# Two mixture-of-experts layers behind an attention: the second x gets a buffer of its own, two groups of transposes move into the first two products, and VectorE makes the token numbers

## The chip, the cores and the metric

The kernel runs on one core of a Trainium2 chip. The metric is the device time of one execution in microseconds (us), and lower is better. TensorE (PE in the profile; PEld are its weight loads) does matrix products, VectorE (DVE), ScalarE (ACT) and GpSimd (POOL) work on elements, SyncE (SP) issues most of the DMAs, and GpSimd issues those that gather or scatter rows by index.

## The reference, cut to what matters

An attention with pooled queries gives 1152 tokens of 512 numbers. They pass two mixture-of-experts layers. Each layer picks one of 8 experts for each token and computes

```python
e_idx = np.argmax(x @ w_gate, axis=1)
gate_w = softmax(x @ w_gate)[arange(N), e_idx]
for e in range(8):
    mask = e_idx == e                       # layer 1: at most `capacity` tokens of an expert
    h = np.maximum(x[mask] @ w1[e], 0.0)    # 512 -> 1024
    y[mask] = gate_w[mask, None] * (h @ w2[e])   # 1024 -> 512
# layer 1: out = y.   layer 2: out = x + y, for tokens with x @ w_skip > 0 only; the others keep x
```

## The kernel before, in words

The code calls the layers m = 0 and m = 1; here they are layer 1 and layer 2. After the attention the x of all tokens lies in device memory (`x_dram`).

**Routing.** VectorE finds each token's expert and its place in a list sorted by expert, cut into tiles of 128 places. The upper and the lower 64 places of a tile may belong to different experts. To turn the places into row indices, VectorE makes `r_tile` (which tile, line 1460) and `r_place` (which place inside, line 1465, three token groups at a time), GpSimd multiplies `r_tile` by the token numbers into `r_ids` (line 651), and TensorE sums the products of `r_place` and `r_ids` (line 892). VectorE writes the result as `rows_in` (line 1473).

**The tiles.** Tile t goes through these steps:

- GpSimd gathers the 128 rows of x into `xraw` (`load_x`, line 601);
- TensorE turns them with 4 transposes (`turn_x`, line 918), ScalarE copies the result to `XT` in two halves (`copy_xt`, line 1154);
- TensorE makes the first product, `hidden_product`: for each of the 4 chunks c of 128 inputs, 4 rows; a row is one matmul of 64 tokens by the expert in the ring `w1ring` (line 931) and, beside it in the other half of the array, one of 64 tokens by `wright` (line 933). `wright` is a copy of the right half's expert, made in four parts by `fill_right` (line 319);
- ScalarE writes relu times gate to `hid` (`relu`, line 1161), TensorE turns it with 8 transposes (`turn_hidden`, also line 918), ScalarE copies to `HT` (line 1169);
- TensorE makes the second product, `y_product`, also 16 rows. VectorE copies the result out, and GpSimd scatters it (line 630).

TensorE's order is written out by hand. A `step(t)` is: first product of t, second product of t - 1, turn x of t + 1, turn hidden of t. In step 0 there is no second product of a tile before, so nothing but the turns stands between first product 0 and first product 1. Here the text calls that stretch the handover. First product 1 writes the same PSUM banks as first product 0, so it waits for relu 0 (`relu_ready`). VectorE refills `wright` for tile 1 when first product 0 is done (`hidden_done`). There are 10 tiles in layer 1 and 9 in layer 2. `keep_busy` are matmuls whose result nobody reads.

Semaphores count what is done: `x_loaded` is raised by 16 by each gather, `x_turned` by 1 for each turned x, `xt_ready` by 1 for each half of `XT`, `w1_right` by 1 for each part of `wright`.

## Time and profile before

| | us |
|---|---|
| median of 3 runs | 610.27 (609.8 to 610.33) |
| the profiled execution | 610.99 |
| its span (first to last instruction) | 608.0 |
| TensorE busy | 589.3 |
| VectorE busy | 313.5 |
| ScalarE busy | 267.1 |
| GpSimd busy | 187.5 |
| attention, from the start to | about 272 |
| routing of layer 1, then its products | 272 to 287.3, then to 442.9 |
| routing of layer 2, then its products | 446 to 460.6, then to 601.2 |

All times below are counted from the start of the span. A row of the timeline shows the start, the duration, the engine, the line, the operation and its operands, and in brackets how long the engine was idle before it and what ended that. When one row holds several instructions ("x4"), the duration is that of all of them.

### The profile page before, as it was taken

The page shows a single profiled execution, that of the slowest core. Times are in us where ns is not written, and L with a number is a line of the kernel's source. Part 1 is how long each engine was busy: PE and PEld are TensorE (multiplying, and loading weights), DVE is VectorE, ACT ScalarE, POOL GpSimd, SP SyncE. Part 2 cuts the span into 40 slices and gives each one's busy share as a digit, 9 for nine tenths or more (in the row PEclk, how much of TensorE's full clock was granted, in tenths as well). Part 3 has the DMA queues.
Part 4 walks back from the last instruction along what each step waited for, and adds up shares of the span by engine and source line. Part 5 has one row for each costly group of instructions (what it writes and reads, how often), then busy time and mean ns, then how long its engine had stood idle before and what let it go on. Part 6 is the DMA issues. An engine that isn't in the chain of part 4 may idle for free.

```text
span 608.0 us, 12473 instructions
## 1 busy us (share of the span) xinstructions
PE 589.3 (97%) x3739; PEld 351.6 (58%) x3740; DVE 313.5 (52%) x658; ACT 267.1 (44%) x440; POOL 187.5 (31%) x164
## 2 busy tenths in 40 slices
PE   8899999999999999999999999999999999999994
PEld 7678787777777877768333333333485333333333
DVE  5457565657566666657324872876674211311111
ACT  4556565556566565530144444444102444444410
POOL 4686534435261900001111121122112022222223
PEclk9999999999999999999999999999999999999998
DMA  8979917262622054002999787890856798951111
GB/s 202 291 176 259 207 41 159 56 142 44 156 47 58 1 160 174 21 12 58 391 415 352 319 315 283 327 322 26 308 183 227 266 314 326 322 180 44 45 52 62
DMA packets 42636, 111.60 MB, mean 184 GB/s; under 512 B 16020, under 2 KB 16020, under 8 KB 41536
## 3 DMA queue, kind: packets, MB, share of 16 engines
q1 hardware_dynamic: 38528, 99.03, 51.4%
q0 software_dynamic: 4080, 12.22, 5.8%
q8 instruction: 15, 0.25, 0.2%
q14 instruction: 13, 0.11, 0.1%
HBM read 102.68 MB, written 12.06 MB: 189 GB/s over the span
## 4 chain that ended last, share of the span: by engine, by line
PE 88%; DVE 4%; issue 3%; DMA 2%; ACT 2%; POOL 1%; DVEq 0%; POOLq 0%; SPq 0%; ACTq 0%
PE psum L931 40%; PE psum L700 15%; PE psum L714 12%; PE psum L748 10%; PE psum L918 4%; PE psum L781 3%; PE psum L760 1%; PE psum L744 1%; DVE probs L1210 1%; ACT probs L1047 1%; DMA qraw<-in_q_dram 1%; PE psum L933 1%; PE psum L839 1%; DMA xraw<-moe_in,rows_in 1%; DMA xraw<-moe_in,idx_x 1%
## 5 line engine op out<-in xcount | busy, mean ns | idle before, releaser
L931 PE MATMUL psum<-w1ring,XT 128*64 x304 | 134.5, 595 | 0.8 <-ACT XT L1154 0.4
L931 PE MATMUL psum<-w2ring,HT 128*64 x336 | 133.7, 552 | 1.6 <-DVE wright L319 1.6
L933 PE MATMUL psum<-wright,XT 128*64 128x512 f32 x304 | 134.5, 595 | 0.0
L933 PE MATMUL psum<-wright,HT 128*64 128x512 f32 (+1 forms) x336 | 133.7, 552 | 0.0
L1210 DVE TENSOR_SCALAR_CACHE_REDUCE probs<-psum 128x1152 f32<-128x1152 f32 x72 | 97.6, 1357 | 62.5 <-PE psum L700 62.5
L1047 ACT ACTIVATE probs<-probs,nmax 128x1152 f32<-128x1152 f32 x72 | 90.7, 1260 | 45.6 <-DVE probs L1210 45.6
L700 PE MATMUL psum<-KT,QT 128*128 128x384 f32 x480 | 101.9, 350 | 3.0 <-DVE probs L1210 1.8
L931 PEld LDWEIGHTS psum<-w2ring,HT 128*64 128x64 f32 x336 | 45.9, 137 | 83.6 <-issue 79.5
L700 PEld LDWEIGHTS psum<-KT,QT 128*128 128x128 f32 x480 | 80.2, 188 | 15.0 <-issue 7.9
L931 PEld LDWEIGHTS psum<-w1ring,XT 128*64 128x64 f32 x304 | 40.1, 137 | 79.8 <-issue 79.8
L714 PE MATMUL psum<-ident,probs 128*128 128x128 f32 x648 | 82.0, 275 | 1.1 <-ACT probs L1047 0.6
L714 PEld LDWEIGHTS psum<-ident,probs 128*128 128x128 f32 x648 | 72.7, 140 | 9.2 <-issue 3.7
L1161 ACT ACTIVATE hid<-psum,slot_gate 128x1024 f32<-128x1024 f32 x19 | 21.2, 1114 | 125.1 <-PE psum L933 125.1
L1054 ACT COPY PT<-psum 128x512 f32<-128x512 f32 x88 | 48.4, 588 | 60.3 <-PE psum L714 60.3
L319 DVE COPY wright<-w2ring 128x1024 f32 x76 | 50.5, 715 | 23.3 <-DMA w2ring<-in_moe_w_dram 23.3
L748 PE MATMUL psum<-PT,V 128*64 128x512 f32 x256 | 62.2, 605 | 0.0
L319 ACT COPY wright<-w1ring 128x1024 f32 x60 | 58.1, 1041 | 0.0
L1389 DVE CUSTOM_DVE_ANT_0 psum<-ysb,wnext 128x512 f32<-128x512 f32 x81 | 52.9, 723 | 3.9 <-DMA wnext<-in_next_w_dram 3.9
L1382 DVE TENSOR_TENSOR orow<-psum,res 128x512 f32<-128x512 f32 x8 | 5.5, 692 | 89.3 <-PE psum L933 89.3
L933 PEld LDWEIGHTS psum<-wright,HT 128*64 128x64 f32 x336 | 45.9, 137 | 0.0
L331 POOL CAST KT<-kraw 128x2304 fp32r<-128x2304 f32 x7 | 14.7, 2107 | 87.2 <-PE psum L700 81.2
L1217 DVE COPY PT<-psum 128x512 f32<-128x512 f32 x56 | 36.4, 687 | 8.3 <-PE psum L714 8.3
(166 smaller groups left out, 602.2 us busy)
## 6 DMA issues: line engine op xcount, KB each, us to landing
w1ring<-in_moe_w_dram SPq DMA_DIRECT2D x64, 512.0 KB, 6.2
w2ring<-in_moe_w_dram SPq DMA_DIRECT2D x64, 512.0 KB
qraw<-in_q_dram SPq DMA_DIRECT2D x30, 288.0 KB, 10.1
kraw<-in_k_dram SPq DMA_DIRECT2D x14, 576.0 KB, 9.1
V<-in_v_dram SPq DMA_DIRECT2D x8, 576.0 KB, 4.0
moe_in<-zero SPq DMA_DIRECT2D x9, 256.0 KB, 3.1
wnext<-in_next_w_dram SPq DMA_DIRECT2D x1, 2304.0 KB, 16.0
out_dram<-moe_in SPq DMA_DIRECT2D x1, 2304.0 KB
```

Of the source, the lines that this page charges most:

```text
L319: copy(wright[k][:, part * PIECE:(part + 1) * PIECE], piece_of(k, slot, part).rearrange("p o f -> p (o f)")).then_inc(filled, 1)
L700: mm = pe.matmul(dst, QT[par][:, piece, q0:q0 + P], KT[par][:, b * S + c * KB:b * S + (c + 1) * KB], start=(i == 0), stop=(i == 2 * len(pa ...
L714: mm = pe.transpose(bank(T_BANK + place % 3)[:, i * P:(i + 1) * P], src, ident[:])
L748: mm = pe.matmul(psum[rows, PV_BANK, :], V[par][:, b * KT_N + j, :], PT[:, j, :], start=(j < 2), stop=False, skip_group_check=True)
L918: return pe.matmul(place[:, chunk * P:(chunk + 1) * P], src, ident[:], is_transpose=True, start=first, stop=False, skip_group_check=True)
L931: pe.matmul(psum[0:GRAIN, b, 0:width], lhs[:, c * P:c * P + GRAIN], left, start=first, stop=last, skip_group_check=True)
L933: return pe.matmul(psum[GRAIN:P, b, 0:width], lhs[:, c * P + GRAIN:(c + 1) * P], wright[k][:, cols], start=first, stop=last, skip_group_ch ...
L1047: nc.scalar.activation(probs[:, t, :], probs[:, t, :], ACT.Exp, bias=nmax[:, t:t + 1], scale=-1.0, accum_out=den[:, t:t + 1]).then_inc(pro ...
L1054: nc.scalar.copy(dst, bank(T_BANK + place % 3, cols)).then_inc(turned_by_act, 1)
L1210: nc.vector.tensor_scalar(probs[:, t, :].rearrange("p (c k) -> p c k", c=3), scores_in(h, t), -SCALE, None, ALU.mult, ALU.min, accum_out=n ...
L1217: nc.vector.tensor_copy(dst, bank(T_BANK + place % 3, cols)).then_inc(turned_by_dve, 1)
L1389: nc.vector.tensor_tensor_reduce(out=bank(JUNK_BANK + e % 2), in0=ysb[:], in1=wnext[:, e, :], scale=1.0, scalar=0.0, op0=ALU.mult, op1=ALU ...
```

## The change

Three things change.

1. `xsecond` is a new buffer for the x of tile 1, with its own semaphore. GpSimd issues its gather right behind that of tile 0. TensorE turns it inside first product 0, behind chunk 1, into the bank of the second product (`turn_second`). VectorE copies it to `XT`, between the parts of `wright`; ScalarE did it before.
2. The 8 transposes of `hid` of tile 0 stand inside first product 1, behind chunk 1, and no longer ahead of it.
3. VectorE makes `r_ids` for the token numbers, between `r_tile` and `r_place`; GpSimd did it before.

The core of the diff:

```diff
+        xsecond = sb_in(moe, "xsecond", [P, DM])
...
+        second_loaded_ = [sem(f"second_loaded_{m}") for m in range(2)]
...
                 def load_x(t, count):
 
-                    wait(pool, x_turned, t)
+                    if not isinstance(t, int) or t > 1:
+                        pool.wait_ge(x_turned, 1 if isinstance(t, int) and t == 2 else t)
                     settle()
                     index = rows_in[m][:, t:t + 1] if isinstance(t, int) else idx_x[:]
+                    into, loaded = (xsecond, second_loaded_[m]) if isinstance(t, int) and t == 1 else (xraw, x_loaded)
...
-                n = ROUTED[m]
-                token = token_id if m == 0 else slot_token
-                pool.wait_ge(tile_ready, m + 1)
-                nc.gpsimd.tensor_tensor(r_ids[:, 0, 0:n, :], r_tile[:, 0:n],
-                                        token[:, 0:n].unsqueeze(2).to_broadcast([P, n, NSLOT]), ALU.mult
-                                        ).then_inc(ids_ready, 1)
                 if m == 0:
                     pool.wait_ge(x_stored, 16 * 4 * H)
                 pool.wait_ge(rows_in_ready, m + 1)
                 load_x(0, 0)
+                load_x(1, 0)
                 pool.wait_ge(tables_ready, m + 1)
                 rest = pool.value_load(tab_n[m][0:1, 0:1], min_val=0, max_val=NSLOT - 2)
-                load_x(1, 0)
                 step(0, first=True)
...
+                def turn_second():
+                    pe.wait_ge(second_loaded_[m], 16)
+                    for c in range(DC):
+                        mm = turn_into(bank(Y_BANK), xsecond[:, c * P:(c + 1) * P], c, c == 0)
+                    mm.then_inc(x_turned, 1)
+
-                def hidden_product(t, place=None):
+                def hidden_product(t, place=None, between=None):
...
+                        if between and c == 1:
+                            between()
                     mm.then_inc(hidden_done, 1)
...
-                step(0, first=own)
-                step(1)
+                hidden_product(0, own, turn_second)
+                pe.wait_ge(gates_found, m + 1)
+                hidden_product(1, None, lambda: turn_hidden(0))
+                y_product(0)
+                turn_x(2)
+                turn_hidden(1)
...
-                    copy_xt(t + 1)
+                    if not isinstance(t, int):
+                        copy_xt(t + 1)
                     copy_hidden(t)
...
-                nc.vector.tensor_tensor(of(r_tile), per_tile(iota_slot, NSLOT), per_slot(r_which), ALU.is_equal
-                                        ).then_inc(tile_ready, 1)
+                tt(of(r_tile), per_tile(iota_slot, NSLOT), per_slot(r_which), ALU.is_equal)
+                token = token_id if m == 0 else slot_token
+                nc.vector.tensor_tensor(r_ids[:, 0, 0:n, :], of(r_tile), per_slot(token), ALU.mult).then_inc(ids_ready, 1)
...
                 dve.wait_ge(hidden_done_[m], START + 1)
-                fill_right(dve, nc.vector.tensor_copy, FIRST, m, *following, w1_right_[m])
+                dve.wait_ge(x_turned_[m], 2)
+                for i in range(2):
+                    cols = slice(i * DM // 2, (i + 1) * DM // 2)
+                    fill_right(dve, nc.vector.tensor_copy, FIRST, m, *following, w1_right_[m], (i,))
+                    nc.vector.tensor_copy(XT[:, cols], bank(Y_BANK)[:, cols]).then_inc(xt_ready_[m], 1)
+                fill_right(dve, nc.vector.tensor_copy, FIRST, m, *following, w1_right_[m], (2, 3))
```

On TensorE, this stood before between the last row of first product 0 and the first row of first product 1 (line 918 are the transposes, line 914 loads the expert's number of the next tile):

```order
L933 MATMUL psum<-wright,XT 64x512
L918 MATMUL psum<-ident,xraw 128x128 x4
L918 MATMUL psum<-ident,hid 128x128 x8
L914 TENSOR_LOAD tab_grain
L914 ISA x2
L946 ISA
L931 REGISTER_ALU
L931 ISA
L931 MATMUL psum<-w1ring,XT 64x512
```

This stands there in the changed kernel (its lines 912, 929, 931 and 950 are 914, 931, 933 and 946 of before):

```order
L931 MATMUL psum<-wright,XT 64x512
L912 TENSOR_LOAD tab_grain
L912 ISA x2
L950 ISA
L929 REGISTER_ALU
L929 ISA
L929 MATMUL psum<-w1ring,XT 64x512
```

Both groups of transposes have left the handover. Where they went reads like this. In the middle of first product 0, around its ninth row, TensorE had before

```order
L931 MATMUL psum<-w1ring,XT 64x512
L933 MATMUL psum<-wright,XT 64x512
L931 ISA
L931 MATMUL psum<-w1ring,XT 64x512
L933 MATMUL psum<-wright,XT 64x512
```

and has now

```order
L929 MATMUL psum<-w1ring,XT 64x512
L931 MATMUL psum<-wright,XT 64x512
L916 MATMUL psum<-ident,xsecond 128x128 x4
L929 ISA
L929 MATMUL psum<-w1ring,XT 64x512
L931 MATMUL psum<-wright,XT 64x512
```

The four transposes of the second x have come in between two rows. The eight of `hid` stand at the same place of first product 1.

On VectorE, at the refill of `wright` for tile 1, this stood before:

```order
L319 REGISTER_ALU
L319 ISA
L319 COPY wright<-w1ring 128x1024
L319 ISA
L319 COPY wright<-w1ring 128x1024
L319 ISA
L319 COPY wright<-w1ring 128x1024
```

and this stands there now:

```order
L321 REGISTER_ALU
L321 ISA
L321 COPY wright<-w1ring 128x1024
L1532 COPY XT<-psum 128x256
L321 ISA
L321 COPY wright<-w1ring 128x1024
L1532 COPY XT<-psum 128x256
L321 ISA
L321 COPY wright<-w1ring 128x1024
```

The first half of `XT` now follows the first part of `wright`, the second half the second part.

## Rows read from the trace of the kernel before

**Rows 1.** The page's chain of work that ended last, by engine.

```profile
PE 88%; DVE 4%; issue 3%; DMA 2%; ACT 2%; POOL 1%; DVEq 0%; POOLq 0%; SPq 0%; ACTq 0%
```

**Rows 2.** Timeline of the handover of layer 1 (start us, us, engine, line, operation).

```profile
293.82 0.59 PE L931 MATMUL psum<-w1ring,XT 128*64 x1
...
294.53 1.11 ACT L1161 ACTIVATE hid<-psum,slot_gate 128x1024 f32<-128x1024 f32 x1 [7.40 <-PE psum L933]
...
294.87 0.63 PE L918 MATMUL psum<-ident,xraw 128*128 128x128 f32 x4 [0.45 <-issue]
294.88 2.50 DVE L319 COPY wright<-w1ring 128x1024 f32 x4 [6.85 <-PE psum L933]
...
295.70 1.09 PE L918 MATMUL psum<-ident,hid 128*128 128x128 f32 x8 [0.20 <-ACT hid L1161]
...
297.07 0.64 PE L931 MATMUL psum<-w1ring,XT 128*64 x1 [0.28 <-issue]
```

**Rows 3.** Timeline of the handover of layer 2.

```profile
467.11 0.59 PE L931 MATMUL psum<-w1ring,XT 128*64 x1
...
467.83 1.11 ACT L1161 ACTIVATE hid<-psum,slot_gate 128x1024 f32<-128x1024 f32 x1 [7.38 <-PE psum L933]
...
468.18 2.50 DVE L319 COPY wright<-w1ring 128x1024 f32 x4 [6.37 <-PE psum L933]
...
468.99 1.09 PE L918 MATMUL psum<-ident,hid 128*128 128x128 f32 x8
...
470.19 0.64 PE L931 MATMUL psum<-w1ring,XT 128*64 x1
```

**Rows 4.** Timeline of TensorE between second product 0 and first product 2.

```profile
310.42 0.59 PE L931 MATMUL psum<-w2ring,HT 128*64 x1
...
310.95 0.66 PE L918 MATMUL psum<-ident,xraw 128*128 128x128 f32 x4
311.44 1.04 PE L918 MATMUL psum<-ident,hid 128*128 128x128 f32 x8
312.41 0.64 PE L931 MATMUL psum<-w1ring,XT 128*64 x1
...
312.89 0.59 PE L931 MATMUL psum<-w1ring,XT 128*64 x1
```

**Rows 5.** Timeline of VectorE in the attention: a copy out of PSUM.

```profile
271.50 0.43 DVE L1230 COPY OT<-psum 128x256 f32<-128x256 f32 x1 [0.54 <-PE psum L744]
```

**Rows 6.** Busy time, granted clock (PEclk) and DMA of the handover of layer 1.

```profile
294.40:297.05 2.65, 1.75 (x14) 1.27 (x12) 2.17 (x4) 2.36 (x5) 0.67 (x1) 1.00 0.99 368
```

**Rows 7.** Routing of layer 1: timeline, and durations (ns, min/median/max) of `r_place`.

```profile
277.73 0.29 DVE L1460 TENSOR_TENSOR r_tile<-iota_slot,r_which 128x126 f32<-128x126 f32 x1
278.19 0.55 POOL L651 TENSOR_TENSOR r_ids<-r_tile,token_id 128x126 fp32r<-128x126 f32 x1 [63.63 <-DVE r_tile L1460]
280.40 0.17 DVE L1473 TENSOR_SCALAR rows_in<-psum 128x14 int32<-128x14 f32 x1
...
L1465 DVE TENSOR_TENSOR r_place<-iota_p,r_inside x3: 545/550/755, 277.9 to 279.1; 128x384 fp32r<-128x384 f32 x3
```

**Rows 8.** The same in layer 2.

```profile
450.80 0.36 DVE L1460 TENSOR_TENSOR r_tile<-iota_slot,r_which 128x196 f32<-128x196 f32 x1
452.06 0.50 PE L892 MATMUL psum<-r_ids,r_place 128*128 128x14 f32 x3 [0.36 <-POOL r_ids L651]
454.52 0.17 DVE L1473 TENSOR_SCALAR rows_in<-psum 128x14 int32<-128x14 f32 x1 [0.81 <-PE psum L892]
...
L1465 DVE TENSOR_TENSOR r_place<-iota_p,r_inside x5: 411/546/876, 451.1 to 453.3; 128x384 fp32r<-128x384 f32 x4, 128x256 fp32r<-128x256 f32 x1
```

**Rows 9.** The first turns of x, and landing times of the gathers of 281 to 298 us.

```profile
285.79 0.65 PE L918 MATMUL psum<-ident,xraw 128*128 128x128 f32 x4 [1.29 <-DMA xraw<-moe_in,rows_in]
459.16 0.60 PE L918 MATMUL psum<-ident,xraw 128*128 128x128 f32 x4
...
DMA to landing us min/median/max: 4.1/7.2/7.4
```

More of the change, by code:

```diff
@@ L197, in build @@
         hot_ready, pos_ready, exp_ready, diff_ready = (sem(n) for n in ("hot_ready", "pos_ready", "exp_ready", "diff_ready"))
-        tile_ready, inside_ready, kept_ready = sem("tile_ready"), sem("inside_ready"), sem("kept_ready")
+        inside_ready, kept_ready = sem("inside_ready"), sem("kept_ready")
         active_ready, ot_part = sem("active_ready"), sem("ot_part")
         ylast_copied, last_logits = sem("ylast_copied"), sem("last_logits")
+        second_loaded_ = [sem(f"second_loaded_{m}") for m in range(2)]
         y_half_, orow_half = [sem(f"y_half_{m}") for m in range(2)], sem("orow_half")
@@ L313, in right_slot, with fill_right @@
             return expert, eng.snap(ring_slot(k, m, expert))
-        def fill_right(eng, copy, k, m, expert, slot, filled):
-            for part in range(PARTS):
+        def fill_right(eng, copy, k, m, expert, slot, filled, parts=range(PARTS)):
+            for part in parts:
                 eng.wait_ge(w_loaded[k][part], expert * 16 + (E * m + 1) * 16)
@@ L601, in load_x @@
                     nc.gpsimd.indirect_dma_start(
-                        out=xraw[:], out_offset=None, in_=x_dram[m],
+                        out=into[:], out_offset=None, in_=x_dram[m],
                         in_offset=bass.IndirectOffsetOnAxis(ap=index, axis=0),
-                        bounds_check=B * SQ - 1, oob_is_err=False).then_inc(x_loaded, 16)
+                        bounds_check=B * SQ - 1, oob_is_err=False).then_inc(loaded, 16)
                 def load_residual(t, count):
@@ L675, in _ @@
                     store_y(rest + 1, done + 1)
-                pool.wait_ge(x_loaded, rest * 16 + 64)
+                pool.wait_ge(x_loaded, rest * 16 + 48)
                 settle()
@@ L921, in turn_x @@
                 def turn_x(t):
-                    pe.wait_ge(x_loaded, 16 * t + 16)
+                    pe.wait_ge(x_loaded, 16 if isinstance(t, int) and t == 0 else 16 * t)
                     wait(pe, xt_ready, 2 * t)
@@ L1011, in next_logits, with step @@
                     mm.then_inc(lg_done, 1)
-                def step(t, first=None):
-                    hidden_product(t, first)
-                    if first:
-                        pe.wait_ge(gates_found, m + 1)
-                    else:
-                        y_product(t - 1)
+                def step(t):
+                    hidden_product(t)
+                    y_product(t - 1)
                     turn_x(t + 1)
@@ L1475, in _ @@
                 tt(r_gcut[:, 1, 0:n], of(gate), r_gcut[:, 0, 0:n].bitcast(F32), ALU.subtract)
-                dve.wait_ge(tile_ready, m + 1)
                 for i in range(2):
```

## The prediction, made before the changed kernel was run

> **What bounds the kernel now.** I read the page first, and there the chain of work that ended last: TensorE holds 88% of it [rows 1], and its busy time is 589.3 us of a span of 608.0 us. So an edit pays only where it takes TensorE's idle time away, and costs wherever it gives TensorE more to wait for. The timeline of the stretches that the change touches comes next. In the steady steps TensorE has no idle time: no row has a bracket [rows 4]. The two handovers, between first product 0 and first product 1 of each layer, do have some. There I count from T, the start of the last row of first product 0.
>
> In layer 1, T is 293.82 and the first row of product 1 starts at 297.07, 3.25 us later [rows 2]. In layer 2 it is 467.11 and 470.19, 3.08 us [rows 3]. Both end the same way: the last row ends at T + 0.6, relu 0 runs to T + 1.82 (294.53 + 1.11 - 293.82), the 8 transposes of `hid` follow it to T + 2.97, and product 1 starts 0.28 us (layer 1) or 0.11 us (layer 2) after them. The 4 transposes of x run while relu does, so they cost nothing there.
>
> The third place is the routing. In layer 1 the first turn of x waits 1.29 us for the gather [rows 9], so whatever delays `rows_in` delays everything behind it. In layer 2 the first turn has no idle time ahead of it [rows 9].
>
> **The change part by part.**
>
> *The transposes inside the products.* Their price is read where TensorE turns without waiting [rows 4]. Rows of a product follow each other every 0.43 us. The first transpose starts 0.53 us after the last row, 0.10 more than a row would; 4 transposes take 0.49 us (310.95 to 311.44), 8 take 0.97 us (311.44 to 312.41); the row behind starts the next one after 0.48 us, 0.05 more. So four inside a product cost 0.10 + 0.49 + 0.05 = 0.64 us, and eight 0.10 + 0.97 + 0.05 = 1.12 us. Together 1.76 us for a layer, all on the path, as a product has no gap to hide them in. The least they can cost is 12 x 0.122 = 1.46 us, if entering and leaving is free; in the other direction I allow 1.9 us, as a mixture of x and `w1ring` rows is not in the trace.
>
> *The handover without transposes.* What is left between the products is the longest of three waits. Relu 0 still has to end, at T + 1.82, since product 1 writes the banks that relu reads. The first part of `wright` has to be copied by VectorE, which starts at T + 1.06 (294.88 - 293.82; 1.07 in layer 2) and takes 2.50 / 4 = 0.63 us for a part. And the first half of `XT` now comes behind that part on VectorE. The copy of 128 x 256 numbers from PSUM took VectorE 0.43 us [rows 5], so it ends at T + 1.06 + 0.63 + 0.43 = T + 2.12. To the first row I add 0.2 us, between the 0.28 and the 0.11 above: T + 2.3. The bounds are T + 1.93 (relu ends last, and 0.11 behind it) and T + 2.7 (the second wait ahead of the copies and the registers of `fill_right` add as much again as the lag). So the handover shrinks from 3.25 to 2.3 us in layer 1 (-0.95) and from 3.08 to 2.3 us in layer 2 (-0.78). The second wait of VectorE, for `x_turned` 2, ends in the middle of product 0 and adds no delay; behind it are queued the parts of `wright` for both products, and TensorE waits for those. The two XT copies push the parts for second product 0 back by some 0.8 us; they are wanted only after the 16 rows of first product 1, 6.9 us, and that covers it. Part 1 of `wright` follows the first XT copy by 0.63 us, and TensorE wants it 4 rows, 1.7 us, later.
>
> The sum of these two is the point of this case: before, relu covered the four x transposes, and the handover held all twelve. Now the handover holds none, but relu and the copies are bare, and the transposes are paid in full elsewhere.
>
> *The gather of the second x.* It goes ahead of the wait for the tables and the register load on GpSimd, and raises a semaphore of its own, so SyncE, which starts the `w2ring` loads when `x_loaded` reaches 16, still waits for the first x alone. Issued about 1.3 us behind the first, it lands at the latest 7.4 us later [rows 9], at about 290.5; its turn stands behind 8 rows of product 0, at 287.4 + 3.4 = 290.8. So it costs nothing, and the gather of the third x takes its old place. On the first x, whose landing took 4.1 us, I count no delay; the bound is the 7.4 us that a gather took beside `w2ring` loads, 3.3 us more.
>
> *Token numbers on VectorE.* In layer 1 `r_ids` comes ahead of `r_place` and costs VectorE what `r_tile` of the same shape takes, 0.29 us, with 0.02 for the link. GpSimd's product ran from 278.19 to 278.74, beside the second `r_place`, and one of the three took 755 ns where the others took about 545 [rows 7]. That 0.21 us comes back. So `rows_in` moves by 0.31 - 0.21 = +0.10 us, and the first x with it; the bounds are -0.1 and +0.31. In layer 2 TensorE waited for GpSimd until 452.06 [rows 8]. Now the first `r_place` would start at 450.80 + 0.36 + 0.02 + 0.28 = 451.46 and take 546 ns: 452.01. So TensorE starts as before, and since VectorE waits for TensorE ahead of `rows_in` there, nothing changes: 0.
>
> The Trainium skill (GPSIMD Engine Reference, Specifications) says that GpSimd's access to SBUF is shared with VectorE, and that VectorE instructions with two SBUF inputs contend with it. The slow `r_place` of each layer, 755 and 876 ns [rows 7, 8], agrees. Without that rule the 0.21 us would be taken for noise, and the sum would be 0.2 us higher.
>
> *The sum.* 2 x 1.76 - 0.95 - 0.78 + 0.10 = +1.89 us. Behind the handovers TensorE goes on without idle time, so it reaches the end. The profiled execution would go from 610.99 (span 608.0 and 2.99 around it) to 612.88; it lies 0.72 us above the median of the runs, 610.27, which gives 612.2.
>
> **The rivals.**
>
> *A: relu bounds the handover, and the switches are free.* If VectorE's copies are done before relu, and entering and leaving a product with transposes costs nothing, a layer pays 1.46 + 1.93 against 3.25 or 3.08: +0.14 and +0.31, with routing at 0 some +0.5 us, 610.8. For it: relu's end at T + 1.82 is only 0.3 us from the copy's. Against it: VectorE started 0.35 us after ScalarE in both layers [rows 2, 3], and the 0.10 us ahead of the first transpose is in the trace [rows 4].
>
> *B: the transposes vanish inside the products (the other side).* The place is the same two products; the price of the twelve would be 0 in place of 1.76, because the page shows weight loads busy for only 58% of the span against TensorE's 97%, and transposes could use what the rows leave. Then the sum is 0.10 - 0.95 - 0.78 = -1.6 us, 608.6. It decides once the twelve cost less than 0.8 us. Against it: the same twelve moved the next row by 1.5 us in the steady steps, where nothing waited [rows 4].
>
> *C: the second gather delays the first.* Both go through the same queue. If the first x landed as late as one beside a weight load, that is +3.3 us in layer 1 and as much in layer 2, at the most 618.8. For it: TensorE does wait for that x [rows 9]. Against it: its data is under way before the second's rows can be, since the issue alone takes over 1 us.
>
> *D: the clock falls.* The granted clock was 1.00, that is 2.4 GHz, over the handover of layer 1, with its pauses and twelve transposes [rows 6]. The changed kernel has one pause of about 1.9 us in place of shorter ones. At 1.2 GHz the 16 rows of product 1 would take 6.9 us more in each layer: up to 626. Against it: nothing in the handovers before made it fall.
>
> **How the numbers follow.** The forecast has a chance of 0.66, A 0.20, B 0.07, C 0.05, D 0.02. The predicted time is 612.2 us. The forecast's own bounds: transposes 1.9, a start at T + 2.5 and routing +0.31 give +2.8, which is 613.0; to A it reaches down to 610.8. With a few tenths for the runs the range is 610.6 to 613.5. A run pair of this kernel can tell about 0.2% from no change, 1.2 us: faster is below 609.05, slower above 611.49. Slower is the forecast, C and D, 0.73; A is the same, 0.20; B is faster, 0.07.
>
> **What would show it.** In the profile of the changed kernel: ninth rows of first products 0 and 1 that start about 1.07 and 1.55 us after the eighth instead of 0.43; a handover of about 2.3 us from T, ended by VectorE's copy of `XT` and not by relu; no idle time ahead of the turn of `xsecond`; all `r_place` near 550 ns, and `rows_in` 0.1 us later in layer 1. A handover under 1.5 us, or inserted transposes under 0.8 us a layer, would make the forecast wrong in sign.

## The result, and the profile after

| | before | changed |
|---|---|---|
| median (us) | 610.03 (609.67 to 610.33, 4 runs) | 614.02 (613.5 to 614.75, 4 runs) |
| ratio, with its 95% interval | | 1.0064 [1.0053, 1.0076] |
| profiled execution, and its span | 610.99, 608.0 | 613.5, 611.7 |
| granted clock, mean of a run | 0.996 or more in the profiled execution and in all 90 runs made beside the experiments | 0.991 to 0.995 |

The change made the kernel 4.0 us slower, twice the forecast of 1.9, and outside the range. The span grew by 3.7 us.

The first view is the timeline of the changed kernel around the handover of layer 1. Lines have moved: the rows of a first product are now L929, the transposes L916, relu L1168, the copies of `wright` L321, the copies of `XT` L1532.

```profile
290.23 0.59 PE L929 MATMUL psum<-w1ring,XT 128*64 x1
...
290.76 0.65 PE L916 MATMUL psum<-ident,xsecond 128*128 128x128 f32 x4
...
291.35 0.64 PE L929 MATMUL psum<-w1ring,XT 128*64 x1
...
291.83 0.59 PE L929 MATMUL psum<-w1ring,XT 128*64 x1
...
294.40 0.59 PE L929 MATMUL psum<-w1ring,XT 128*64 x1
...
295.11 1.11 ACT L1168 ACTIVATE hid<-psum,slot_gate 128x1024 f32<-128x1024 f32 x1 [8.17 <-PE psum L931]
295.46 0.69 DVE L321 COPY wright<-w1ring 128x1024 f32 x1 [7.22 <-PE psum L931]
296.07 0.42 DVE L1532 COPY XT<-psum 128x256 f32<-128x256 f32 x1
...
296.95 0.64 PE L929 MATMUL psum<-w1ring,XT 128*64 x1 [1.95 <-DVE XT L1532]
...
298.29 1.06 PE L929 MATMUL psum<-w1ring,XT 128*64 x1
...
299.14 1.06 PE L929 MATMUL psum<-w1ring,XT 128*64 x1
```

This answers to [rows 2]. The handover runs from 294.40 to 296.95: 2.55 us, where it was 3.25. It is ended by VectorE's copy of `XT`, as forecast. No idle time stands ahead of the turn of `xsecond`, so its gather came in time. The first turn of x starts no later than before (below): rival C is out. The four transposes push the ninth row from 290.66 (0.43 behind the eighth) to 291.35, and the tenth follows 0.48 later: 1.12 + 0.48 - 0.86 = 0.74 us for the four. The last two rows show what the forecast had set aside: rows of product 1 that last 1.06 us in place of 0.59 and follow each other every 0.85 us in place of 0.43. The windows of the same stretch say why. Their columns are those of [rows 6]; the granted clock is the third number from the right.

```profile
294.50:297.00 2.50, 0.55 (x6) 0.06 (x2) 1.54 (x3) 1.11 (x1) 0.00 (x0) 1.00 1.02 410
297.00:299.00 2.00, 2.00 (x8) 0.70 (x10) 2.00 (x5) 0.00 (x0) 0.00 (x0) 0.82 1.03 356
299.00:301.00 2.00, 2.00 (x8) 0.65 (x6) 1.43 (x3) 0.00 (x0) 0.00 (x0) 0.50 0.96 305
301.00:303.00 2.00, 2.00 (x13) 0.87 (x10) 0.69 (x1) 0.03 (x1) 0.00 (x0) 0.83 0.97 365
```

Behind the pause of 1.95 us TensorE still had 1.00, that is 2.4 GHz, for its first three rows, and then 0.50, 1.2 GHz, from about 298.3 until about 301.7. The clock that was not granted is 2.00 x 0.18 + 2.00 x 0.50 + 2.00 x 0.17 = 1.7 us. [rows 6] had 1.00 over its handover, and the profile of before has 1.00 in the same place of the product too.

In layer 2 the handover looks the same (answer to [rows 3]), and the eight transposes inside first product 1 can be read without a change of clock.

```profile
470.33 0.59 PE L929 MATMUL psum<-w1ring,XT 128*64 x1
...
472.88 0.64 PE L929 MATMUL psum<-w1ring,XT 128*64 x1 [1.96 <-DVE XT L1532]
...
475.93 0.59 PE L929 MATMUL psum<-w1ring,XT 128*64 x1
...
476.47 1.10 PE L916 MATMUL psum<-ident,hid 128*128 128x128 f32 x8
...
477.50 0.64 PE L929 MATMUL psum<-w1ring,XT 128*64 x1
...
477.98 0.59 PE L929 MATMUL psum<-w1ring,XT 128*64 x1
```

The handover is 2.55 us again. The eight cost 1.57 + 0.48 - 0.86 = 1.19 us. Here the rows behind the pause keep their 0.43 us.

The routing answers to [rows 7] and [rows 8]. First comes the timeline of VectorE in layer 1 with the first turn of x (answer to [rows 9]), then the durations of `r_place` in layer 2.

```profile
278.07 0.29 DVE L1470 TENSOR_TENSOR r_ids<-r_tile,token_id 128x126 fp32r<-128x126 f32 x1
278.28 1.49 DVE L1474 TENSOR_TENSOR r_place<-iota_p,r_inside 128x384 fp32r<-128x384 f32 x3
...
280.54 0.17 DVE L1482 TENSOR_SCALAR rows_in<-psum 128x14 int32<-128x14 f32 x1
...
285.60 0.66 PE L916 MATMUL psum<-ident,xraw 128*128 128x128 f32 x4 [0.96 <-DMA xraw<-moe_in,rows_in]
```

```profile
L1474 DVE TENSOR_TENSOR r_place<-iota_p,r_inside x5: 419/551/552, 453.9 to 455.7; 128x384 fp32r<-128x384 f32 x4, 128x256 fp32r<-128x256 f32 x1
```

No `r_place` is slow any more (three took 1.49 us in layer 1), and `rows_in` comes 0.14 us later than before. The first gather landed a little sooner, so that the first turn starts at 285.60 against 285.79.

One more difference lies ahead of the routing of layer 2. VectorE's copy of `logits` there starts at 448.55 against 445.78, 2.77 us later; `r_held`, which waits for TensorE's counts, at 451.57 against 449.18, 2.39 later. These are its rows, before and then changed; the idle time ahead of it is 0.56 and 0.18.

```profile
449.18 0.17 DVE L1444 TENSOR_SCALAR r_held<-psum 128x8 f32<-128x8 f32 x1 [0.56 <-PE psum L868]
```

```profile
451.57 0.17 DVE L1452 TENSOR_SCALAR r_held<-psum 128x8 f32<-128x8 f32 x1 [0.18 <-PE psum L866]
```

The trace gives the sum: transposes 2 x (0.74 + 1.19) = +3.86; handovers (2.55 - 3.25) + (2.55 - 3.08) = -1.23; an earlier first product in layer 1, -0.16 (287.18 against 287.34); 0.28 us given back by the start of the products of layer 2 (a delay of 2.48 us there against 2.76 at second product 0 of layer 1); 0.22 us given back at the last second product, ahead of which TensorE waited 0.65 us in place of 0.95 (a start at 597.62 against 593.96, 3.66 us later, where the delay had been 3.88 at second product 0 of layer 2); low clock +1.7. Together +3.7, and the span grew by 3.7.

### The profile page after: what moved, and what is told of

It is laid out like the page before. It is cut to its first block, busy times and chain, and to the rows that moved or that the text cites. A ratio compares the mean times of both kernels' runs of the same rounds, so it can differ in the third digit from the quotient of the medians.

```text
span 611.7 us, 12468 instructions
## 1 busy us (share of the span) xinstructions
PE 590.8 (97%) x3739; PEld 351.2 (57%) x3740; DVE 314.8 (51%) x664; ACT 265.9 (43%) x436; POOL 185.0 (30%) x162
## 4 chain that ended last, share of the span: by engine, by line
PE 88%; DVE 5%; issue 3%; ACT 1%; DMA 1%; DVEq 1%; POOL 1%; POOLq 0%; SPq 0%
PE psum L929 41%; PE psum L698 14%; PE psum L712 12%; PE psum L746 9%; PE psum L916 4%; PE psum L779 3%; PE psum L758 1%; PE psum L837 1%; PE psum L742 1%; DVE probs L1218 1%; ACT probs L1054 1%; PE psum L931 1%; DMA qraw<-in_q_dram 1%; DVE wright L321 1%; POOL out_dram L634 0%
## 5 line engine op out<-in xcount | busy, mean ns | idle before, releaser
L929 PE MATMUL psum<-w1ring,XT 128*64 x304 | 137.0, 602 | 4.4 <-DVE XT L1532 3.9
L931 PE MATMUL psum<-wright,XT 128*64 128x512 f32 x304 | 137.1, 602 | 0.0
L929 PE MATMUL psum<-w2ring,HT 128*64 x336 | 133.7, 552 | 1.3 <-ACT HT L1176 0.6
L929 PEld LDWEIGHTS psum<-w2ring,HT 128*64 128x64 f32 x336 | 45.9, 137 | 83.1 <-issue 79.1
L929 PEld LDWEIGHTS psum<-w1ring,XT 128*64 128x64 f32 x304 | 40.1, 138 | 84.0 <-issue 84.0
L1168 ACT ACTIVATE hid<-psum,slot_gate 128x1024 f32<-128x1024 f32 x19 | 21.2, 1115 | 119.3 <-PE psum L931 119.3
L321 DVE COPY wright<-w2ring 128x1024 f32 x76 | 50.1, 711 | 18.4 <-DMA w2ring<-in_moe_w_dram 18.4
L321 ACT COPY wright<-w1ring 128x1024 f32 x60 | 58.1, 1041 | 0.0
L634 POOL DMA_INDIRECT moe_in<-ysb,idx_y x9 | 10.6, 1179 | 99.6 <-DVE ysb L1387 99.6
```

The lines of the kernel that those rows point to most:

```text
L321: copy(wright[k][:, part * PIECE:(part + 1) * PIECE], piece_of(k, slot, part).rearrange("p o f -> p (o f)")).then_inc(filled, 1)
L929: pe.matmul(psum[0:GRAIN, b, 0:width], lhs[:, c * P:c * P + GRAIN], left, start=first, stop=last, skip_group_check=True)
L931: return pe.matmul(psum[GRAIN:P, b, 0:width], lhs[:, c * P + GRAIN:(c + 1) * P], wright[k][:, cols], start=first, stop=last, skip_group_ch ...
L1168: nc.scalar.activation(hid[:].rearrange("p (c f) -> p c f", c=2), psum[:, HID_BANK:HID_BANK + 2, :], ACT.Relu, scale=g).then_inc(relu_read ...
```

## The experiments

"The change" is the changed kernel. Every ratio is to the kernel before on the same chip, with its 95% interval.

**e1_routing**: the kernel before, with only the routing part of the change.

```
-                pool.wait_ge(tile_ready, m + 1)
-                nc.gpsimd.tensor_tensor(r_ids[:, 0, 0:n, :], r_tile[:, 0:n], ...)
+                nc.vector.tensor_tensor(r_ids[:, 0, 0:n, :], of(r_tile), per_slot(token), ALU.mult).then_inc(ids_ready, 1)
```

> The kernel before with the third part of the change alone: VectorE makes the token numbers. Theory: the two traces differ at the start of first product 0 by -0.16 us in layer 1 and in the routing of layer 2 by -0.28 us, both from this part, so the time falls by 0.3 to 0.5 us (ratio about 0.9993). Rival: those were the landing time of one gather and one wait of VectorE that happened to be short, and the time is that of before within 0.1 us. In both, r_place takes about 550 ns everywhere.

Measured: 0.9999 [0.999, 1.0008], 610.23 us. All full-sized `r_place` took 551 to 553 ns, as in the change, and yet the time is that of before; the interval leaves room for 0.6 us either way. The profile is sharper. From `r_tile` to `rows_in` layer 1 took 2.80 us, where before took 2.67 and the change 2.80. In layer 2 VectorE's wait ahead of `r_held` was 0.56 us, as before, and not the 0.18 of the change. So the routing part does not bring the 0.28 us given back, and it costs well under a microsecond.

**e2_kept_busy**: the change, with `keep_busy(6)` in the handover: six calls of two short products of `ident` each, so "x12" in the profile.

```
                 hidden_product(0, own, turn_second)
                 pe.wait_ge(gates_found, m + 1)
+                keep_busy(6, X_BANK)
                 hidden_product(1, None, lambda: turn_hidden(0))
```

> The changed kernel with 6 idle matmul calls (12 rows of 0.12 us, 1.5 us) in the handover between first product 0 and first product 1, where TensorE stood still for 1.95 us. Theory: that pause makes the granted clock fall behind it, in layer 1 of the changed kernel from about 298 to 301.7 us, 1.7 us lost a layer where it happens. With the pause filled the clock stays at 1.00, and the time is that of before plus 2.2 us (two handovers at 2.55 us, transposes in the products at 1.93 us a layer, routing -0.4). Rival: the clock falls for another reason (the transposes inside the products, or chance), and the time stays at that of the changed kernel, before plus 3.9 us, with the low clock still in the trace.

Measured: 1.0043 [1.003, 1.0055], 612.48 us, granted clock 0.996 or 0.997 in all 6 runs. The timeline of its handover in layer 1:

```profile
295.05 0.59 PE L929 MATMUL psum<-w1ring,XT 128*64 x1
...
295.58 1.60 PE L837 MATMUL psum<-ident 128*128 128x128 f32 x12
...
296.72 0.42 DVE L1533 COPY XT<-psum 128x256 f32<-128x256 f32 x1
...
297.60 0.64 PE L929 MATMUL psum<-w1ring,XT 128*64 x1 [0.41 <-DVE XT L1533]
```

The handover is 2.55 us as in the change, but TensorE stands idle for 0.41 us of it instead of 1.95. The work put in computes nothing, and yet the kernel is faster than the change: by 1.3 us if the ratios of this run and of the first result are compared (1.0043 against 1.0064), by 0.7 us against e5 (1.0055), with intervals that overlap. The clock tells it more clearly than the time. None of the 6 runs is at 0.995 or less, where 7 of the 10 runs of the change are (e5 below); if the filling did nothing, so uneven a split would come about once in 100 times. The expectation was +2.2 us for a clock that stays up, and +2.4 came. Two of the 6 runs took 613.6 and 613.7 us at a clock of 0.997; what delayed those isn't shown.

**e3_hid_back**: the change, with the eight transposes of `hid` back in the handover; those of x stay inside product 0.

```
                 pe.wait_ge(gates_found, m + 1)
-                hidden_product(1, None, lambda: turn_hidden(0))
+                turn_hidden(0)
+                hidden_product(1, None)
```

> The changed kernel with the 8 transposes of hid of tile 0 back in the handover; the second x is still turned inside first product 0. Theory: the handover ends as before, about 3.1 to 3.2 us after the last row (relu 1.85, transposes 1.1, first row 0.1 to 0.3), and TensorE stands still for 1.4 us at a time at the most, so the clock stays up. Before plus 2 x 0.74 for the turn of x, minus 0.4 for routing: +1.0 to +1.1 us. Rival: the transposes inside first product 0 make the clock fall, and it is +2.7 us or more, with a low clock behind the handover.

Measured: 1.002 [1.0011, 1.0029], 611.38 us, clock 0.996 or more in all 11 runs.

```profile
294.81 0.59 PE L929 MATMUL psum<-w1ring,XT 128*64 x1
...
296.78 1.06 PE L916 MATMUL psum<-ident,hid 128*128 128x128 f32 x8 [1.37 <-ACT hid L1169]
...
298.13 0.64 PE L929 MATMUL psum<-w1ring,XT 128*64 x1 [0.28 <-DVE XT L1533]
```

The handover is back at 3.32 us (3.17 in layer 2), no shorter than before: moving x alone out of it frees nothing, because relu and the eight transposes fill it. The four transposes inside the product are a pure cost, 2 x 0.74. With +0.07 and +0.09 for the handovers, and the 0.16 and 0.28 of the sum above taken off, that makes 1.2 us, where 1.3 was measured (611.38 against 610.06). The gains taken off are those of the change's profile; in the profile of e3 they are smaller in front (0.04 and 0.15) and 0.29 at the last second product. The longest pause is 1.37 us and no run has a low clock.

**e4_x_back**: the other half undone: x is turned in the handover, `hid` inside product 1. VectorE's waits are those of the change.

```
-                hidden_product(0, own, turn_second)
+                hidden_product(0, own)
                 pe.wait_ge(gates_found, m + 1)
+                turn_second()
                 hidden_product(1, None, lambda: turn_hidden(0))
```

> The changed kernel with the turn of the second x in the handover; the 8 transposes of hid are still inside first product 1. Theory: the turn fits into the time in which TensorE waits for relu and VectorE, so the handover stays at 2.55 us and product 0 loses its 0.74 us: before plus 2 x 1.19 - 0.70 - 0.53 - 0.4, +0.7 us, and the clock stays up as the pause is cut in two pieces below 1.4 us. Rival: the transposes inside first product 1 make the clock fall, and it is +2.4 us or more. If the pause of 1.4 us is still enough for a fall, it is +2.4 us as well, but then e3 falls too.

Measured: 1.005 [1.0036, 1.0065], 613.45 us, clock 0.994 to 0.997. The expectation was wrong, and the timeline shows why:

```profile
295.26 0.59 PE L929 MATMUL psum<-w1ring,XT 128*64 x1
...
296.97 0.69 DVE L321 COPY wright<-w1ring 128x1024 f32 x1 [7.34 <-PE psum L916]
297.58 0.42 DVE L1533 COPY XT<-psum 128x256 f32<-128x256 f32 x1
...
298.46 0.64 PE L929 MATMUL psum<-w1ring,XT 128*64 x1 [2.01 <-DVE XT L1533]
```

VectorE waits for the turned x ahead of all its copies, the first part of `wright` too. With the turn in the handover that wait ends late, and the copies start at T + 1.71 instead of T + 1.06. The handover becomes 3.20 us with a pause of 2.01 us. Five of the 6 runs have a clock of 0.994 or 0.995. In the profiled one the fall was elsewhere, in the opening of the attention, behind a pause of 1.98 us that is 0.72 us in the kernel before and 1.53 in the change; behind both handovers, with pauses of 2.01 us, the clock stayed at 1.00. So the five low runs can't all be put down to the handover. That some are is likely, and not shown: the opening is the same code in all kernels, and the kernel before had no low clock in 90 runs. The row of the opening, and the window behind it:

```profile
10.23 6.05 PE L698 MATMUL psum<-KT,QT 128*128 128x384 f32 x24 [1.98 <-DVE KT L1355]
```

```profile
12.00:24.00 12.00, 10.67 (x65) 9.90 (x63) 6.33 (x10) 7.26 (x11) 7.30 (x5) 0.88 1.02 249
```

**e5_change_again**: the change once more.

> The changed kernel once more, on the same chip as the next three, as the measure of how often its clock falls. Theory (the unbroken pause of 1.95 us in the handover makes the clock fall): mean granted clock of most runs at 0.991 to 0.995 against 0.996 to 0.999 before, and a time of before plus 3.5 to 4.5 us. Rival (chance): clocks like those of before in most runs, and plus 2.6 us as with the pause filled.

Measured: 1.0055 [1.0042, 1.0068], 613.34 us, in two groups: 612.0, 612.27, 612.63 us with a clock of 0.997 or 0.998, and 614.05, 614.12, 614.24 us with 0.994 or 0.995. Its profiled run is of the first group. The pause is there, the fall is not:

```profile
297.19 0.64 PE L929 MATMUL psum<-w1ring,XT 128*64 x1 [1.95 <-DVE XT L1532]
```

```profile
297.00:299.00 2.00, 1.81 (x10) 0.70 (x12) 2.00 (x5) 0.00 (x0) 0.00 (x0) 1.00 0.92 344
299.00:301.00 2.00, 2.00 (x12) 0.63 (x9) 1.66 (x3) 0.00 (x0) 0.00 (x0) 1.00 0.98 320
```

So the pause makes a fall possible and not certain. Against the 610.16 us of before on this chip the change costs 1.8 to 2.5 us without it and 3.9 to 4.1 with it.

**e6_x_back_mended**: e4 with VectorE's first copy ahead of its wait for the turned x.

```
                 dve.wait_ge(hidden_done_[m], START + 1)
-                dve.wait_ge(x_turned_[m], 2)
                 for i in range(2):
                     ...
                     fill_right(dve, nc.vector.tensor_copy, FIRST, m, *following, w1_right_[m], (i,))
+                    if i == 0:
+                        dve.wait_ge(x_turned_[m], 2)
```

> As the run with the turn of the second x in the handover, but VectorE copies the first part of wright before it waits for that turn. Theory: the handover comes back from 3.20 to 2.55 us, as in the changed kernel, since the wait for the turn stood ahead of all of VectorE's work; with it before plus 2 x 1.19 - 0.70 - 0.53, +1.2 us, and the clock stays up because the longest pause is 1.4 us. Rival: the handover was long for another reason and stays at 3.2 us; or the clock falls here too, and it is +2.9 us or more.

Measured: 1.0006 [0.9997, 1.0015], 610.68 us, clock 0.996 or more in 11 runs. A twelfth took 866.85 us at a clock of 0.654; it is left out, and what disturbed it is not known.

```profile
293.68 0.59 PE L929 MATMUL psum<-w1ring,XT 128*64 x1
...
295.34 0.42 DVE L1534 COPY XT<-psum 128x256 f32<-128x256 f32 x1
...
296.22 0.64 PE L929 MATMUL psum<-w1ring,XT 128*64 x1 [1.36 <-DVE XT L1534]
```

The handover is 2.54 us with the turn of x inside it. That is the change's own length, so in the change the four transposes of x were moved out of a place where they cost nothing. The pause is 1.36 us, and none of the 11 runs has a low clock. The time missed the forecast: +0.5 us came, not +1.2. The sum of the expectation left out what its profile gives back as the change's does: 0.28 us by the start of the products of layer 2, and 0.30 at the last second product.

**e7_split_relu**: both turns in the handover, x from its own buffer; relu 0 in two halves, the first half started when the first of its two PSUM banks is complete; `XT` by ScalarE as before; the registers for product 1 read ahead of the turns.

```
+                    if isinstance(t, int) and t == 0:
+                        act.wait_ge(half_hidden_[m], 1)
+                        nc.scalar.activation(hid[:, 0:512], bank(HID_BANK), ...).then_inc(relu_half_[m], 1)
+                        act.wait_ge(hidden_done, START + 1)
+                        nc.scalar.activation(hid[:, 512:1024], bank(HID_BANK + 1), ...).then_inc(relu_ready, 1)
...
+                second = hidden_place(1)
+                turn_second()
+                turn_hidden(0)
+                hidden_product(1, second)
```

> The kernel that the traces point to: the gather of the second x is early and into its own buffer, but both groups of transposes stand in the handover as before; the number of the next expert is read ahead of them, and relu of tile 0 is split in two, so that its first half runs beside the last two rows of first product 0. Theory: relu is what holds the handover. The first half of relu is done about T + 0.5, four transposes of x run to T + 1.0, eight of hid to T + 2.0, where XT by ScalarE (T + 1.7) and the first part of wright (T + 1.7) are ready: a handover of 2.1 us and no transposes elsewhere, -1.15 and -1.0 us, together -2.1 us. Rival: wright and XT hold it (they did at 2.55 us in the changed kernel), 2.4 to 2.6 us, and it is -1.1 to -1.4 us.

Measured: 1.0012 [0.9993, 1.0032], 611.03 us, again in groups: four of the 12 runs at 608.0 to 608.1 us with a clock of 0.996 to 0.998, six at 610.87 to 613.34 with 0.989 or 0.99, and two at 609.43 and 611.2 with 0.997. In the profiled run, one of the four, the handovers took 2.34 and 2.17 us, where 2.1 was expected, and the four are 2.1 us faster than before, as the theory had it. The median is not: the low clock took the gain away.

**e8_early_place**: e7 without the split of relu.

> The same without the split of relu. Theory: relu ends at T + 1.85, eight transposes to T + 2.9, product 1 starts about T + 3.0 in both layers: -0.25 and -0.1 us, -0.3 us against before, which is at the edge of what five rounds can tell. Rival: the gather of the second x, which in the kernel before landed 0.9 us after the last row had started, held the handover; then the gain is 0.5 us a layer.

Measured: 1.0016 [0.9996, 1.0036], 610.15 us. Eight of 12 runs lie at 609.5 to 610.8, one at 611.93, and three with a clock of 0.988 to 0.992 stand at 613.75 to 616.51. The median of the other nine is 609.76, 0.4 us below before, where 0.3 was expected. The profiled run is one of the three. Its handovers took 2.90 us with a pause of 0.68 or 0.69 us at a clock of 1.00; against e7 that shows the split of relu at work, with 0.56 and 0.73 us. The fall is in the routing of layer 2:

```profile
456.00:459.00 3.00, 3.00 (x18) 3.00 (x18) 2.52 (x12) 0.00 (x0) 1.56 (x2) 0.58 0.05 15
459.00:462.00 3.00, 3.00 (x15) 3.00 (x15) 2.02 (x4) 0.00 (x0) 1.99 (x3) 0.50 0.50 165
462.00:465.00 3.00, 2.93 (x21) 2.73 (x19) 1.43 (x6) 0.65 (x2) 0.17 (x1) 0.78 0.77 180
```

Ahead of it, from 450 us to 456 at a clock of 1.00, TensorE did only short products, with one pause:

```profile
453.68 0.47 PE L890 MATMUL psum<-r_ids,r_place 128*128 128x14 f32 x3 [0.47 <-DVE r_place L1477]
```

The clock not granted is 3 x 0.42 + 3 x 0.50 + 3 x 0.22 = 3.4 us. This is a second place where the clock can fall. That the pause of 0.47 us is its cause is not shown: the clock was still at 1.00 for 2.8 us behind it, until 456.5, and the same pause stands in the profiles of e1, e7, e10 and e12, where nothing fell.

**e9_split_busy** and **e10_split_again**, on one chip: e7 with 17 calls of two short products instead of 13 in both routings, and e7 unchanged.

```
-                keep_busy((13, 13)[m], HID_BANK + 1)
+                keep_busy((17, 17)[m], HID_BANK + 1)
```

> The kernel with both turns back between products 0 and 1 (from xsecond, relu 0 in two halves), and 17 instead of 13 short products of ident ahead of the routing's product of r_ids and r_place, in both layers, so that TensorE's pause of 0.47 us there is covered. Theory: the clock falls that hit over half of the runs of the split version begin in the routing (as in the profile of the version without the split, where the granted clock was 0.50 from 459 us on, behind that pause of 0.47 us): with the pause filled, the median is near the clean runs, ratio 0.9965 to 0.9975 (some 608.2 us), the granted clock of all runs 0.996 or more. Rival 1: the fall has nothing to do with that pause (the same pause stands in kernels without falls): runs spread as before, 608 to 613 us, clock down to 0.989 in some, ratio 0.999 to 1.002. Rival 2: the four more short products delay the products behind them by some 0.1 to 0.3 us a layer: ratio 0.998 with a clean clock.

> The split version once more, unchanged, on the same chip. If its falls of the clock are a property of the kernel, runs near 608 us and runs of 611 to 613 us with a granted clock of 0.99 come again, about half and half. If they were a matter of that chip or that time, all runs are near 608 us (ratio 0.9965) with a clock of 0.996 or more. A profile with a fall would show in which stretch it lies: the theory says the routing of layer 2 or the end of layer 1, since the fillings before product 1 pass in it with pauses under 1.4 us.

Measured: e9 0.999 [0.9981, 0.9999], 609.27 us, clock 0.995 or more in 11 runs. e10 0.9964 [0.9951, 0.9978], 608.12 us, clock 0.996 or more in its 5 runs. e10 had no falls on this chip, so the pair can't tell whether the filling prevents them. It does tell the price, and it is more than the second rival had: e9 is 1.1 us slower than e10. In its profile `rows_in` comes 0.75 us later behind `r_tile` than in e10's in layer 1, where there was no pause to fill, and 0.20 us later behind the logits in layer 2.

The profiled run of e10 is its slowest, 610.63 us, and it had no low clock (0.997). It lost its time in layer 1, ahead of the second product of tile 2, where TensorE waited 2.49 us for VectorE's copy of `wright`, and VectorE for the load of `w2ring`:

```profile
336.10 0.64 PE L930 MATMUL psum<-w2ring,HT 128*64 x1 [2.49 <-DVE wright L322]
```

```profile
335.00:337.00 2.00, 0.90 (x4) 0.35 (x6) 1.34 (x2) 2.00 (x3) 0.00 (x0) 1.00 1.03 420
337.00:339.00 2.00, 2.00 (x12) 0.74 (x10) 0.69 (x1) 1.72 (x2) 0.18 (x1) 1.00 1.03 420
```

So a run can be 2.5 us longer without any fall of the clock. And this pause, longer than that of the change, was followed by a clock of 1.00.

**e11_split_filled** and **e12_split_third**, on one chip: e7 with 15 such calls in layer 2 alone, and e7 unchanged. (Where the expectation of e12 has 7 low-clock runs of 12, e7 had six: those at 0.989 or 0.99.)

```
-                keep_busy((13, 13)[m], HID_BANK + 1)
+                keep_busy((13, 15)[m], HID_BANK + 1)
```

> The split version with 15 instead of 13 short products of ident ahead of the routing's product of r_ids and r_place, in layer 2 alone (there TensorE paused 0.47 us; in layer 1 it did not pause). Each of these products took 0.22 us, so two of them fill 0.44 us of the pause of 0.47 us and delay nothing. Theory (the falls begin at that pause): all runs near 608 us, ratio 0.9965, granted clock 0.996 or more in all. Rival (the falls have another place, or come by chance with a chip): some of the runs at 611 to 613 us with a clock near 0.99, as the unfilled version may show in the same call.

> The split version unchanged, for comparison on the same chip. It gave 7 low-clock runs of 12 in one call and none of 5 in another. If it shows them here and the filled version does not, the filling is what removes them; if neither shows them, this call cannot tell.

Measured: e11 0.9979 [0.9966, 0.9991], 608.35 us, one of 12 runs with a low clock (0.994, 612.22 us). e12 0.9984 [0.9971, 0.9997], 608.62 us, two of 12 (0.99 and 0.989, at 611.18 and 612.35 us). One against two of 12 is no difference. Both are some 0.2% faster than the kernel before, with intervals below 1; e7, the same kernel as e12, was not (1.0012). The handover of e12 in layer 1:

```profile
293.58 0.69 ACT L1180 ACTIVATE hid<-psum,slot_gate 128x512 f32<-128x512 f32 x1 [6.57 <-PE psum L932]
293.74 0.59 PE L930 MATMUL psum<-w1ring,XT 128*64 x1
...
294.27 0.66 PE L917 MATMUL psum<-ident,xsecond 128*128 128x128 f32 x4
...
294.38 0.69 ACT L1183 ACTIVATE hid<-psum,slot_gate 128x512 f32<-128x512 f32 x1
...
294.76 1.04 PE L917 MATMUL psum<-ident,hid 128*128 128x128 f32 x8
...
295.91 0.64 PE L930 MATMUL psum<-w1ring,XT 128*64 x1
```

From T to product 1 are 2.17 us, with all twelve transposes inside and no bracket on TensorE: the handover is now as long as its transposes, and relu and the copies go on beside them. That is 1.08 us less than in [rows 2], and 0.38 us less than the handover that the change emptied. In the profiles of e7 and e11 it is 2.34 us in layer 1, with 0.27 us of "issue" ahead of product 1.

## Why the prediction was wrong, step by step

**The mechanism was right.** Moving work out of a handover that relu and the copies bound anyway, into a product without gaps, costs more than it gives. e6 shows it for x most plainly (2.54 us with the turn, 2.55 without it), e3 for the x part alone (+1.2 us).

**The transposes inside the products** were put at 0.64 and 1.12 us and took 0.74 and 1.19: +3.86 where +3.52 was forecast. Entering was read rightly (the first transpose starts 0.53 or 0.54 us after the row), and so was the row behind the first row after them (0.48). What came short lies between the first transpose and the next row: 0.59 us for four (290.76 to 291.35) where 0.49 was read, and 1.03 for eight (476.47 to 477.50) where 0.97 was read. In [rows 4] the four of x are followed by other transposes and not by a row, so their way back to a row stood nowhere in that reading; why the eight took 0.06 more is open. The forecast's bound of 1.9 us a layer was 0.03 short of the 1.93.

**The handover without transposes** was put at T + 2.3 and was T + 2.55 in both layers: -1.23 where -1.73 was forecast. The end of the `XT` copy was right (T + 2.12 forecast, T + 2.09 measured). What failed is "to the first row I add 0.2 us". Those 0.28 and 0.11 of [rows 2, 3] lay behind TensorE's own transposes. Behind VectorE's copy of `XT` the lag is 0.46 us, and it is that in the change, e2, e4 and e6 alike. It isn't the price of every wait for VectorE: behind the copy of [rows 5], which ended at 271.93, the product that waited for it started at 272.07. What fills the 0.46 us was not separated.

**The routing** was put at +0.10 us, by a later `rows_in` in layer 1. That term was right: from `r_tile` to `rows_in` the change and e1 take 2.80 us, +0.13. The whole part is too small for the time of e1 to show, [0.999, 1.0008]. The Trainium skill (GPSIMD Engine Reference, Specifications) has VectorE instructions with two SBUF inputs contend with GpSimd. The trace agrees, since without GpSimd's product all `r_place` of full size took some 550 ns where one took 755 and one 876.

**What was not in the sum.** First, the first product of layer 1 came 0.16 us sooner, in place of 0.10 later. That hangs on when the first gather lands: TensorE waited for it between 0.90 and 1.48 us in the profiles of the changed kernels, so this gain is luck of the run. Second, 0.28 us were given back at the routing of layer 2, where VectorE waited 0.38 us less for TensorE's counts. That is no chance: the wait is 0.18 us in the profiles of the change, e2, e3, e4, e5 and e6, in all of which VectorE copies the second `XT`, and 0.56 in those of before, e1 and e7 to e12, in which ScalarE does. Why is open. Third, 0.22 us were given back at the last second product; the shorter wait there, 0.65 in place of 0.95 us, is in all kernels with the early second gather but e8, and its cause is open too.

These steps make 1.89 + 0.34 + 0.50 - 0.26 - 0.28 - 0.22 = +2.0 us. e5 shows +1.8 to +2.5 in its runs without a fall (612.0 to 612.6), and e2 +2.4 with the pause filled. That the forecast of 612.2 lies so near those runs is in part luck: the transposes and the handovers were 0.84 us too cheap, and 0.76 us of gains that the forecast had not made up for most of it.

**The clock, rival D, was the step that failed.** Without it the time would have been inside the range. It was given a chance of 0.02 with the argument that "nothing in the handovers before made it fall". But the handovers before had TensorE idle for 0.45, 0.20 and 0.28 us at a time [rows 2] (0.53 at the most in layer 2), and the same text had already worked out that the changed one would have "one pause of about 1.9 us in place of shorter ones". A trace in which no such pause occurs is no evidence on what one does. The price was off the other way: the rival took all 32 rows at 1.2 GHz (up to 626), where the fall ended after some 3.4 us and cost 1.7. With a fall of this size in one layer the sum becomes +3.7 us, the growth of the span.

The runs by the longest pause of TensorE in the handovers of the profiled run, and how many of them had a clock of 0.995 or less:

| kernel | pause, us | low-clock runs |
|---|---|---|
| before | 0.53 | 0 of 90 |
| e1 | 1.05 | 0 of 11 |
| e2 | 0.42 | 0 of 6 |
| e6, e3 | 1.36, 1.37 | 0 of 22 |
| the change, twice | 1.96 | 7 of 10 |
| e4 | 2.01 | 5 of 6 |
| e8 | 0.69 | 3 of 12 |
| e7, e10, e12 (one kernel) | 0.27 or less | 8 of 29 |
| e9, e11 | 0.27 or less | 2 of 23 |

That the pause brings the fall in the change rests on two things: in its profile the fall stands right behind the pause, and e2, which fills the pause and leaves the rest, has no low run. In which stretch the other low runs of the change lost their time is not on record. The pause alone does not decide: it was followed by a fall in one of the four handovers of 1.95 or 1.96 us that were profiled, by none behind the two of 2.01 us in e4, and by none behind the 2.49 us in e10. And the lower rows of the table are falls without a long handover: e8 shows one in the routing. The kernel of e7, e10 and e12 had 6 of 12, 0 of 5 and 2 of 12 low runs; in which stretch is open, because every profile of that kernel fell on a run without one.

## What to carry to other kernels

In this kernel the gap in which TensorE waits for another engine was the cheapest place for its small work. Before moving work out of such a gap, ask what ends it once it is empty. To shorten it, start the engine that bounds it sooner, as the split relu did. And where an edit joins short pauses into one long one, price the clock as a term of its own, with runs repeated, since one profile shows only one of the two outcomes.

## What the runs showed of the hardware that was not expected

- A pause of 1.95 us was followed by 1.2 GHz for about 3.4 us in one profiled execution and by 2.4 GHz throughout in another of the same program; none of the 22 runs of the two kernels with handover pauses of 1.36 and 1.37 us had a low clock. In e10 a pause of 2.49 us was followed by 2.4 GHz. The Trainium skill (TensorE: Matmul & The Clock Gate, HAM oscillation — how this bites in real kernels) tells of a kernel that was throttled at each wait between its groups of products. The trace agrees for the wait of layer 1 in the profile of the change, and not for the equal wait of layer 2 beside it, 1.96 us, behind which the rows kept 0.43 us.
- The clock also fell in the routing, while TensorE did short products (e8), at a cost of 3.4 us. The pause of 0.47 us ahead of it stands in four other profiles, with no fall.
- A kernel with twelve more products that compute nothing in each of two handovers was not slower but 0.7 to 1.3 us faster (e2 against the change, by their ratios to before).
- TensorE's first row started 0.46 us behind the end of VectorE's copy of `XT` in four kernels, and 0.11 to 0.28 us behind its own transposes.
- In one profile TensorE waited 2.49 us in the middle of layer 1 for VectorE's copy of weights that had landed late. It is the profile of a kernel (e10) whose other profiles, e7 and e12, show no wait there; that run was 2.5 us longer at full clock.
